# Zero matmuls on TensorE during the first attention of a fused attention and MLP kernel

## What is computed

```python
for t in range(S):
    m_new = np.maximum(f_gate[:, :, t] + m, i_gate[:, :, t])
    f_stab = np.exp(f_gate[:, :, t] + m - m_new)
    i_stab = np.exp(i_gate[:, :, t] - m_new)
    m = m_new
    C = f_stab * C + i_stab * einsum('bhd,bhe->bhde', vt, kt)
    n = f_stab * n + i_stab * kt
    y[:, :, t] = sigmoid(o_gate_t) * (C @ qt) / max(|n . qt|, 1)
```

## Time and profile before

| what | us |
|---|---|
| runs shown: lowest, median, highest | 302.97, 303.89, 305.05 |
| profiled execution, its own time | 303.86 |
| its span, first to last instruction | 302.0 |
| PE busy in the span | 270.7 (90%) |
| DVE busy | 203.2 (67%) |
| ACT busy | 122.6 (41%) |
| POOL busy | 88.0 (29%) |

### The profile page before, as it was taken

The page is one execution under the profiler, slowest core; times in us unless marked ns, Lnnn a source line. Parts: engine busy times, 40 slices in busy tenths (PEclk is TensorE's granted clock), DMA queues, the critical chain, the costliest instruction groups (busy, mean ns, idle before and its releaser), DMA issues.

```text
span 302.0 us, 5376 instructions
## 1 busy us (share of the span) xinstructions
PE 270.7 (90%) x2024; PEld 258.9 (86%) x2024; DVE 203.2 (67%) x415; ACT 122.6 (41%) x225; POOL 88.0 (29%) x102
## 2 busy tenths in 40 slices
PE   0689678759999999999999999999999999999875
PEld 0577567659989999999899999999999999999774
DVE  7989999785698667866776521534674048762693
ACT  2656465226945453254333222432223333222623
POOL 4435755650066554324500400000012000040440
PEclk9959979796999999999999999999999999999979
DMA  7599964515567235322000001000000100000011
GB/s 219 159 305 306 294 178 123 174 30 208 173 161 243 77 90 150 88 80 67 0 0 3 0 22 46 0 2 0 0 3 0 64 4 0 2 0 1 24 43 65
DMA packets 26289, 25.70 MB, mean 85 GB/s; under 512 B 13976, under 2 KB 22008, under 8 KB 26264
## 3 DMA queue, kind: packets, MB, share of 16 engines
q1 hardware_dynamic: 21976, 18.72, 21.2%
q10 hardware_dynamic: 4288, 6.64, 6.8%
HBM read 23.34 MB, written 2.02 MB: 84 GB/s over the span
## 4 chain that ended last, share of the span: by engine, by line
PE 62%; DVE 10%; ACT 4%; issue 3%; DMA 2%; POOL 2%; ACTq 0%; DVEq 0%; POOLq 0%
PE shared L1177 25%; PE h_ps L1315 18%; DVE prob L939 3%; PE shared L1280 2%; PE s_ps L1215 2%; PE s_ps L1252 2%; PE shared L1265 2%; PE hv_ps L1196 2%; PE hv_ps L1200 1%; DMA stage<-val 1%; PE s_ps L1436 1%; DVE y_lo L948 1%; PE h_ps L1252 1%; PE shared L1284 1%; POOL x L628 1%
## 5 line engine op out<-in xcount | busy, mean ns | idle before, releaser
L1107 DVE SCALAR_TENSOR_TENSOR h_lo<-shared,h_hi 128x384 fp32r<-128x384 f32 x48 | 26.4, 557 | 35.0 <-ACT h_hi L831 34.8
L1315 PE MATMUL h_ps<-ch_hi,h_hi 128*128 128x320 f32 x144 | 45.4, 315 | 0.0
L831 ACT ACTIVATE h_hi<-shared 128x384 fp32r<-128x384 f32 x48 | 23.2, 489 | 53.5 <-PE shared L1177 50.7
L1315 PE MATMUL h_ps<-ch_hi,h_lo 128*128 128x320 f32 x144 | 44.5, 309 | 0.0
L1315 PE MATMUL h_ps<-ch_lo,h_hi 128*128 128x320 f32 x144 | 44.3, 308 | 0.0
L1177 PE MATMUL shared<-u_hi,ch_hi 128*128 128x384 f32 x96 | 32.9, 342 | 0.6 <-DVE yt L988 0.3
L1177 PE MATMUL shared<-u_lo,ch_hi 128*128 128x384 f32 x96 | 32.5, 339 | 0.0
L1177 PE MATMUL shared<-u_hi,ch_lo 128*128 128x384 f32 x96 | 32.5, 339 | 0.0
L1215 PE MATMUL s_ps<-q_in,k_in 128*128 128x128 f32 x192 | 27.5, 303 | 3.6 <-DMA q_in<-qT 3.5
L1215 PEld LDWEIGHTS s_ps<-q_in,k_in 128*128 128x128 f32 x192 | 25.6, 214 | 5.5 <-DMA q_in<-qT 4.2
L1043 DVE SCALAR_TENSOR_TENSOR gate<-x,conv_sb,gate 128x384 f32<-128x384 f32 x44 | 29.0, 667 | 1.0
(11 more groups left out here) (191 smaller groups left out, 636.6 us busy)
## 6 DMA issues: line engine op xcount, KB each, us to landing
G_all<-G_scratch SPq DMA_DIRECT2D x11, 512.0 KB, 5.0
o_sig<-on ACTq DMA_DIRECT2D x2, 960.0 KB, 6.0
k_in<-kT SPq DMA_DIRECT2D x24, 80.0 KB
q_in<-qT SPq DMA_DIRECT2D x24, 80.0 KB
kn_in<-kn SPq DMA_DIRECT2D x12, 160.0 KB, 4.3
v_in<-vn SPq DMA_DIRECT2D x12, 160.0 KB, 4.8
stage<-ch ACTq DMA_DIRECT2D x3, 640.0 KB, 4.3
out<-o_sb SPq DMA_DIRECT2D x12, 160.0 KB, 1.8
```

The lines of the kernel that those rows point to most:

```text
L831: act.activation(h_hi[i % 3][:], ps_of(key)[:, 0:T], ACT.Relu).then_inc(hi_ready, 1)
L1107: took(dve.scalar_tensor_tensor(out=h_lo[i % 3][:], in0=ps_of(key)[:, 0:T], scalar=0.0, in1=h_hi[i % 3][:].bitcast(F32), op0=ALU.max, op1= ...
L1315: last = pe.matmul(h2_ps[t][:, 0:DM], a[:, tile_cols(t)], w[:, f, :], start=(f == 0 and n == 0), stop=(f == FT - 1 and n == 2))
```

## The change

A tile `idle` of 128x512 fp32r is placed in memory that is free then, and DVE zeroes it as its first instruction. PE gets a helper, `keep_warm(times)`, that multiplies it with itself into `h2_ps[0]`, 512 columns each, with no one waiting for the outcome. PE runs 10 of these as soon as the zeroing is done, ahead of `columns(0)`, 7 behind `columns(0)`, and 6 behind the delta of each of the chunks 0 to 3: 41 in all. In the order of PE the groups of 6 stand ahead of `columns(1)` (chunk 0) and ahead of `turn_y(0, n)` (chunks 1 to 3).

```diff
+        idle = sb("idle", [P, HG * L], F32R, at=a_at + 4 * S + 4 * 2 * HG * L)
...
+            dve.memset(idle[:].bitcast(F32), 0.0).then_inc(idle_ready, 1)
             dve.memset(k_in[0][:], 0.0).then_inc(zeroed, 1)
             dve.memset(q_in[0][:], 0.0).then_inc(zeroed, 1)
...
                     last.then_inc(shared_full, 1)
+                    if u < 4:
+                        keep_warm(6)
...
+            def keep_warm(times):
+
+                for _ in range(times):
+                    pe.matmul(h2_ps[0][:], idle[:, 0:P], idle[:], start=True, stop=True)
+
+            pe.wait_ge(idle_ready, 1)
+            keep_warm(10)
             pe.wait_ge(ident_ready, 1)
             columns(0)
+            keep_warm(7)
             for n in range(ATT_STEPS):
                 attention(0, n)
```

More of the change, by code:

```diff
@@ L177, in build @@
         reset = sb("reset", [B * H, S], at=a_at)
+        idle = sb("idle", [P, HG * L], F32R, at=a_at + 4 * S + 4 * 2 * HG * L)
+        assert a_at + 4 * S + 4 * 3 * HG * L <= spot[0]
         taps = [sb(f"taps{k}", [P, T], at=a_at + 4 * T * k) for k in range(KW)]
@@ L274, in build @@
         ident_ready = sem("ident_ready")
+        idle_ready = sem("idle_ready")
         o_ready = sem("o_ready")
```

## The result

| kernel | median us | executions | ratio to before, 95% interval |
|---|---|---|---|
| before, beside the changed one | 304.39 | 302.97 to 305.05 | |
| changed | 308.23 | 308.17 to 308.85 | 1.0133 [1.0106, 1.016] |
| changed, once more on another chip | 307.41 | 305.53 to 308.41 | 1.0082 [1.0055, 1.0109] |

The change makes the kernel slower, by 2.5 to 4 us. The forecast was 304.2 with 306.0 as its upper end. The two profiled executions are 303.86 and 308.85 us, and their spans 302.0 and 307.1.

The account below looks back on a forecast made before the run. The prediction took DVE, POOL where they meet, and the loads to bound the first attention, not PE. Its terms, 0.37 + 0.1 - 0.1 = +0.4 us on 303.86, gave 304.2 us, range 302.2 to 306.0.

Parts of the forecast that it names:

- What bounds the kernel: First attention: the path runs over DVE, POOL where they meet, and the loads; not over PE until 55 us or so.
- The zeroing, +0.37 us: Kernel start: zeroing moves DVE by 0.58 us, a load wait takes up 0.21; the scans and later loads move 0.37.
- The first 17 matmuls, 0: Around columns(0): scores of chunk 0 start up to 1.0 us later, then 1.7 us shorter; hidden, 0 us.
- Six behind delta of chunk 0: +0.1, bound 0.6: Ahead of columns(1): it ends between 17.3 and 18.5 us; hidden or up to 0.6 us, taken as 0.1.
- Six behind the deltas of chunks 1 to 3: +0.1: Ahead of turn_y: chunk 1 about even, +0.2 us; chunks 2 and 3 cost 0; taken together +0.1.
- What the holds take up: First attention: POOL holds DVE until 31.1 and 38.2 us, so delays from the groups of six are hidden there.
- the stated bound with nothing taken up: Groups of six, if the holds take up no delay: 0.6 + 0.2 + 1.1 = 1.9 us.
- The zero matmuls are in the way: Rival, chance 0.15: zero matmuls delay columns(1) and turn_y by up to 3.1 us, 307.0; 305.5 likelier.
- three places: Chunks 0, 1 and 2, where the groups of six were to cost 1.1, about 1.6 and up to 1.1 us.
- The clock stays up where PE is on the path: Rival, chance 0.17: the low clock at 56.28 us goes, giving 302.6; if that at 66.52 goes too, 299.2.

Follow-up runs that it names:

- all_gap_filled: The changed kernel with 16 more zero matmuls behind the scores of chunk 0, where PE idles; 303.76 us, ratio to before 0.9991.
- apart_on_act: The kernel before with batch 0's copies of the state made by ACT instead of DVE; 296.26 us, ratio to before 0.9731.
- zeroing_only: The changed kernel without any of its 41 zero matmuls, the tile still zeroed by DVE; 304.67 us, ratio to before 0.9987.
- fill_54_64_286: The kernel before with idle matmuls in three waits of PE: 7 at 53.8 us, 14 at 63.7, 13 near 286; 303.66 us, ratio 0.9979.
- start_only: The changed kernel without the groups of six, keeping the zeroing and the 17 matmuls around columns(0); 304.54 us, ratio to before 0.998.
- after_again: The changed kernel unaltered, run once more beside the kernel before on another chip; 307.41 us, ratio to before 1.0082.
- twelve: The changed kernel with 12 zero matmuls in each group instead of 6; 308.39 us, ratio to before 1.015.
- after_apart_on_act: The changed kernel with batch 0's copies of the state made by ACT instead of DVE; 298.72 us, ratio to before 0.9823.

## Why the prediction was wrong

Step by step, as it was put.

*What bounds the kernel.* Right. DVE and its meetings with POOL set the first attention, and PE's clock there is worth nothing: all_gap_filled holds full clock to 32 us and gains nothing, and apart_on_act takes the meetings away and gains 8 us.

*The zeroing, +0.37 us.* Over-sized. The first scan started at 3.51 instead of 3.26, so +0.25, and the time of zeroing_only is not told apart from before (0.9987). The load that the term hangs on, `G_all`, isn't steady enough to show it: DVE's wait for it ends at 18.09 before, at 18.49 in fill_54_64_286, which doesn't zero the tile either, and at 19.13 in zeroing_only.

*The first 17 matmuls, 0.* Right: they ran from 1.45 to 8.5 us, the scores took 2.05 us as priced, and start_only is not slower.

*Six behind delta of chunk 0: +0.1, bound 0.6.* This failed. The fall was expected at about 15.3 us, inside the six. It came at 13.73, ahead of delta, so that delta (1.22 us instead of 0.76), all six (2.93, priced 1.4 to 2.6) and the transposes behind them (0.69 for the last five) ran at half clock. `columns(1)` ended at 19.81, not between 17.3 and 18.5, and the exponents of chunk 1 started 2.3 us later than before. Delta at half clock and the transposes had no price at all.

*Six behind the deltas of chunks 1 to 3: +0.1.* This failed at chunk 1, first by its premise on the clock: "From the delta of chunk 0 on PE is now busy without a break, so the clock should be up before 22.13". It rose at 23.97 though PE was busy in 9.40 of 10.22 us. So the scores of chunk 1, which started 2.6 us later, took 3.17 us, where they were to end about 1 us earlier than before; `turn_y` came at 26.89 instead of 23.15, and the wait of 1.62 us stands where +0.2 was put. In after_again the fall came at 15.53, where it was expected, and the rise at 22.36; the exponents of chunk 2 were still 2.2 us late (27.00 against 24.82) and the kernel 3 us slower. So it isn't only that execution's clock. Chunks 2 and 3 did cost nothing, as said. (The sum also has a single +0.1 for the two groups of terms, and takes off 0.1 for a shorter wait at chunk 1, where the term itself has a longer one; that is 0.1 or 0.2 us of it.)

*What the holds take up.* At the exponents of chunk 2 the terms so far are 3.7 us in the trace, against 0.37 + 0.1 + 0.2 = 0.67 forecast, so that even the stated bound with nothing taken up, 1.9 us for all groups, was too small. On top of that the prediction had a delay hidden behind POOL. POOL's operations were treated as if they stood at fixed times, 31.1 and 38.2 us, up to which a late DVE loses nothing. But POOL's chain in a step starts with `y`, which waits for DVE's `yt`. The timeline of POOL in the changed kernel:

```profile
28.66 0.86 POOL L608 TENSOR_TENSOR y<-yt,o_sig 128x320 f32<-128x320 f32 x1 [5.65 <-DVE yt L992]
...
30.45 0.46 POOL L586 TENSOR_TENSOR kept<-state,decay 104x164 f32<-104x164 f32 x1
...
32.10 1.84 POOL L542 TENSOR_TENSOR tok_lo<-stage,tok_hi 128x768 fp32r<-128x768 f32 x1
```

`yt` came 3.7 us later and POOL moved with it: `y` from 24.98 to 28.66, and the `tok_lo` of 29.33 is at 32.10. The hold moved with what it was to hide, and the copies of chunk 2, short before, were held for 3.73 us. It hides only what is late between `yt` and itself, which is why the groups of chunks 2 and 3, behind `yt` of their step, cost nothing even at twelve, and do cost without the holds (after_apart_on_act). The prediction named the load of `v` as what starts POOL; that is so only while the load is later than `y`.

*The rivals.* "The zero matmuls are in the way" had 0.15 and is what happened in the main, with 307.0 as its full price against 308.23 and 307.41 measured. Two of its three places are those of the trace, `columns(1)` and `turn_y` of chunk 1, both dearer than put. The third, chunk 2, cost no wait, and its condition, half clock in all of chunks 0 to 2, was met only up to the scores of chunk 1. That the total lies near its price is luck in part. "The clock stays up where PE is on the path" had its sign: the fall at 56.28 is gone and the wait before the last `den` is short, in the timeline of DVE of the changed kernel:

```profile
63.65 0.17 DVE L982 TENSOR_SCALAR den<-shared 128x8 f32<-128x8 f32 x1 [0.43 <-PE shared L1242]
```

That is 1.6 us less than before, but zeroing_only has the same short wait without a zero matmul, so it isn't shown that the change gave it back. The loss ahead of it is larger in any case.

## What to carry to other kernels

A dummy matmul is work in the engine's order, and where it was meant to cure a low clock here it was paid at the low clock (2.93 us for six, against 1.65). It belongs into a wait that is longer than it, with nothing behind it that another engine waits for, and only where the profile shows that engine on the path; a full clock beside the path is worth nothing. Before a delay is booked as hidden behind another engine's work, ask what starts that work: if it is started by the engine that is late, it moves along.

## What the runs showed of the hardware

- Matmuls on zeros raise the granted clock like others: its first recorded rise is at 4.4 to 7.1 us in the nine traces with the early 17, and at 11.2 to 12.9 in the five without them that have one before 20 us.
- The same kernel's clock falls and rises at other places from one execution to the next: the first low stretch is 13.73 to 23.97 us in one trace of the changed kernel and 15.53 to 22.36 in the other. One trace before gave me the place of a fall as if it were the kernel's own.
- DVE's two copies of the state take 0.48 us at 89 us, 0.9 in some chunks of batch 0, and 3.7 to 4.2 when a row of POOL's operations has just begun. For chunk 2 a start from 0.04 us ahead of POOL's `wv` to 0.01 behind it went with 0.93 us in three traces, one of 0.1 to 0.8 behind with 3.7 to 4.2 in twelve.
